# Moved places in the loads and sums, and the order P6, P2, P7, P5 in two groups of an attention and MLP kernel

## The chip, the cores and the metric

One Trainium2 chip, one of its cores. The time is the device time of one execution in microseconds, the median of several executions. The order of work is written out by hand for each engine: SP issues all DMA, TensorE multiplies, ScalarE (ACT), VectorE (DVE) and GpSimd (POOL) prepare operands and empty the accumulators, and semaphores join them.

## What is computed

Four batches of 8 heads, 576 tokens and 64 columns per head. Windowed attention gives x (2304 tokens x 512), a mix of rank 32 over the tokens is added to it, then comes a two layer network with a residual, then a gated layer:

```python
attn = softmax(scale * q @ k.T + bias, window 128) @ v      # per head, joined to x
u  = x + (x.T @ U @ V).T                                    # rank 32 over tokens
x2 = u + relu(u @ w_ch1) @ w_ch2                            # 512 -> 2048 -> 512
h  = relu(x2 @ w_in); a, v = halves of h                    # 512 -> 1024
out = (a * (w_spatial @ norm(v) + b_spatial)) @ w_out       # 512 -> 512
```

## The kernel before

All products are fp32 by parts: each operand is split into a high and a low part (`hi_...` on ScalarE writes a rounded copy, `lo_...` on VectorE or GpSimd the difference), and three matmuls per tile are summed.

The two large products are done block-wise with seven products instead of eight (2 x 2 blocks, sums of blocks as operands). The products are P1 to P7; P1 has blocks 11, P2 blocks 12 and 21, P6, P7, P4 and P5 sums of blocks, P3 a sum on the weights' side. The **up** product (u @ w_ch1) runs in 24 units s = 0 to 23, eight for each of three groups of 768 tokens; in unit s TensorE does P1, P4 and P3 of the unit before, P2, P6, P5, P7 (list `UP`). Of these, `keep_p` on ScalarE copies P1, P6 and P7 to `sums_u`, and `c11`, `c12`, `c22` (VectorE) and `c21` (ScalarE) make the four result blocks, which `store_r` writes to `r_scr`. P3 of a unit can start when `c22` has read P5's bank. At u = 0 and u = 7 of a group, the operands of the next group are made: `x_sum` (sums of blocks of u, on VectorE), `hi_xs` and `lo_xs` (the two parts, `xs`). TensorE needs them in the order 1, 2, 6, 5, 7, 4, 3.

The **down** product (relu(...) @ w_ch2) is a list of 84 entries n (`ENTRIES`): 3 groups g, 7 products, 4 quarters j. Before, the order in each group is P1, then P3 and P4 of the group before, then P2, P6, P5, P7. A ring of three places `rk` holds the operand: `hi_r(n)` on ScalarE waits until entry n - 3 has been used, `lo_r(n)` on VectorE follows, TensorE then does 12 matmuls of 128x384. `r_sum(g, t, j)` on VectorE makes the sums for P7 (t = 3), P6 (t = 2), P4 (t = 4), P5 (t = 1), 16 per group, at places given by the tables `FIRST_T` (group 0) and `NEXT_T`. They read the relu blocks a, b, c, d, which SP reads back from `r_scr` (`load_raw`, `next_raw`). After P1, P6 and P7 ScalarE copies the banks (`keep_dp`) and VectorE adds the residual (`add_res`); `dc` adds P2 (11), P3 (12) and P5 (22), `dc21` adds P4.

VectorE's list over n is, in this order: what ended three entries ago by P2, P3 or P4 gets its `dc`; what ended four entries ago by P1, P6 or P7 gets its `add_res`; and

```python
                if n > RING + 1 and ENTRIES[n - RING - 2][1:] == (7, DP - 1):
                    dc(ENTRIES[n - RING - 2][0], 22)
                lo_r(n)
```

with `dc(g, 22)` waiting for `rk_used` of all of P5 of group g; then the `r_sum` of entry n.

GpSimd splits attention outputs (`lo_x`, tile `xl`) and weights (`split_wc`), and makes the four sums of W1's second pair (`w1_sum_1`, tile `wst`). From the first group change on it makes and splits W2's sums (`split_w2(kk)`, kk = 0 to 7), as soon as the last `lo_xs` of group 1 is done; SP loads them by `W2_LOAD` and stores them by `W2_STORE`, each at a unit s. SP works in strict order, so an issue that waits holds all behind it. The mix of batch 0 (`mix_down`) needs `xl` of pairs 0 to 3.

Of the kernel before, what the change touches and what calls it, by code (L numbers as in the profile page):

```python
# [38 lines left out]
G = 3  # L39
# [46 lines left out]

DN = []
for _g in range(G):
    DN += [(_g, 1)] + ([(_g - 1, 3), (_g - 1, 4)] if _g else []) + [(_g, m) for m in (2, 6, 5, 7)]
# [6 lines left out]
W2_LOAD = {7: [0, 1], 9: [2], 10: [3], 11: [4], 12: [5], 15: [6], 16: [7]}  # L96
# [8 lines left out]
FIRST_T = {(2, 1): [(3, 0), (2, 0)], (2, 2): [(3, 1), (2, 1)], (2, 3): [(3, 2), (2, 2)], (6, 0): [(3, 3), (2, 3)],  # L105
           (6, 1): [(4, 0), (1, 0)], (6, 2): [(4, 1), (1, 1)], (6, 3): [(4, 2), (1, 2)], (5, 0): [(4, 3), (1, 3)]}
NEXT_T = {(4, 1): [(3, 0)], (4, 2): [(3, 1)], (4, 3): [(3, 2), (2, 0)], (2, 0): [(3, 3), (2, 1)], (2, 1): [(2, 2)],
          (2, 2): [(2, 3)], (2, 3): [(4, 0)], (6, 0): [(1, 0), (4, 1)], (6, 1): [(1, 1), (4, 2)],
          (6, 2): [(1, 2), (4, 3)], (6, 3): [(1, 3)]}


def program(nc, qk, v_n, mu, mv, w1, w2, w_in, w_sp, b_sp, w_out, out_t, u_scr, r_scr, w2_scr, x2_scr, wc_scr):
    ctx = ExitStack()
    with ctx:
# [282 lines left out]
        def _(sp):  # L397
# [167 lines left out]
            for p in range(PAIRS, (B - 1) * PAIRS):  # L565
                load_qk(*divmod(p, PAIRS))
                load_v(*divmod(p - 1, PAIRS))
                prepare(p)
            load_qk(B - 1, 0)
# [13 lines left out]
            load_w1(2)  # L583
# [33 lines left out]
            sp.wait_ge(up_p, UP_AT[(NU - 1, 3)])  # L617
# [3 lines left out]
            store_r(NU - 1)  # L621
            load_w2q(5)
# [15 lines left out]
            for g in range(1, G):  # L638
# [10 lines left out]
                if g == G - 1:  # L649
# [3 lines left out]
                    load_group(range(0, WU))  # L653
                store_x2(g, 11)
                if g < G - 1:
                    next_raw(g + 1, "a", 0)
                load_u(g, 21)
                if g < G - 1:
                    next_raw(g + 1, "a", 1)
                    next_raw(g + 1, "b", 0)  # L660
                    next_raw(g + 1, "b", 1)
            sp.wait_ge(rk_lo, ENTRY[(G - 1, 5)] + DP)
            for n in x2_out:
                sp.wait_ge(x2_out[n], 16 * (2 if n != 11 else 3))
            load_x2(0, slice(0, 2), x2_first[0])
            sp.wait_ge(rk_lo, ENTRY[(G - 1, 7)] + DP)
            load_x2(0, slice(2, 3), x2_first[1])
# [6 lines left out]
            sp.wait_ge(rk_used, DN_AT[(G - 1, 7)])  # L674
# [21 lines left out]
        def _(pool):  # L696
# [161 lines left out]
            for p in range(1, (B - 2) * PAIRS + 2):  # L858
# [3 lines left out]
                if p == 2:  # L862
# [34 lines left out]
        def _(act):  # L897
# [227 lines left out]
            for n in range(RING, len(ENTRIES)):  # L1125
# [8 lines left out]
                if g == G - 1 and j == 0 and m == 3:  # L1134
                    act.wait_ge(rk_used, DN_AT[(G - 1, 6)])
# [74 lines left out]
        def _(dve):  # L1210
# [295 lines left out]
            for s in range(1, NU):  # L1506
# [14 lines left out]
                if u == 0:  # L1521
                    lo_xs(g, 5)
                    lo_xs(g, 4)
# [5 lines left out]
                c11(s)  # L1529
                if u == UNITS - 1 and g < G - 1:  # L1530
# [554 lines left out]
```

## Time and profile before

| | us |
|---|---|
| median of 3 runs | 742.55 (742.05 to 748.79) |
| profiled execution, device time | 744.08 |
| its span, first to last instruction | 742.3 |
| TensorE matmuls busy | 721.9 |
| VectorE busy | 455.4 |
| ScalarE busy | 339.3 |
| GpSimd busy | 182.4 |

The profile is of one execution. Its times count from the first instruction. Up products run from 153.3 to 346.6, down products from 340.4 to 525.9 (the last up products lie between its first entries), then the gated layer to the end. Busy TensorE means that a matmul is in flight; matmuls of 384 columns follow each other every 0.173 us. A row of the timeline gives start, duration, engine, line, operation, and in brackets how long the engine stood idle before it and what ended that.

### The profile page before, as it was taken

What the parts mean: (1) busy time and instruction counts of PE and PEld (TensorE: products, weight loads), DVE (VectorE), ACT (ScalarE), POOL (GpSimd) and SP (SyncE); (2) the same over time, 40 slices, a digit from 0 to 9 for tenths busy, and PEclk for the clock granted to TensorE, in tenths of its full rate; (3) what the DMA queues carried; (4) which work ended last, traced back from release to release, by engine and by line L of the source; (5) the groups of instructions that cost most, each with busy time, mean ns of one, the idle gap of its engine ahead of it and who ended that gap; (6) DMA issues with size and microseconds to landing.
All of it is one profiled execution on the core that took longest, in us unless ns stands there. A gap on an engine that the chain in (4) does not pass through costs nothing.

```text
span 742.3 us, 13178 instructions
## 1 busy us (share of the span) xinstructions
PE 721.9 (97%) x4688; PEld 665.2 (90%) x4688; DVE 455.4 (61%) x1032; ACT 339.3 (46%) x764; POOL 182.4 (25%) x183
## 2 busy tenths in 40 slices
PE   8989999989999998999999999999999999999998
PEld 5767777779999998999899999999899998998997
DVE  6858686888855256325977965975466435444431
ACT  5967778855443234224344444444252432432422
POOL 1596645420005884326050000000010100100100
PEclk9999999999999999999999999999999999999999
DMA  6668875045465766797995354645940100100101
GB/s 205 187 236 308 293 261 175 16 142 170 150 216 199 286 245 220 281 346 296 422 304 192 117 167 148 216 163 166 357 167 1 49 17 0 64 0 0 64 0 64
DMA packets 74066, 128.24 MB, mean 173 GB/s; under 512 B 5024, under 2 KB 44960, under 8 KB 73504
## 3 DMA queue, kind: packets, MB, share of 16 engines
q1 hardware_dynamic: 74016, 127.59, 49.7%
q8 instruction: 29, 0.48, 0.3%
q14 instruction: 21, 0.17, 0.1%
HBM read 76.91 MB, written 50.66 MB: 172 GB/s over the span
## 4 chain that ended last, share of the span: by engine, by line
PE 79%; DVE 12%; issue 3%; POOL 2%; ACT 2%; DMA 1%; SPq 0%; DVEq 0%; ACTq 0%; POOLq 0%
PE bank L1862 7%; PE bank L1864 7%; PE bank L1863 7%; PE bank L1704 3%; PE bank L1904 3%; PE wide L1719 3%; PE bank L1905 3%; PE bank L1906 3%; PE bank L2013 2%; PE bank L2015 2%; PE bank L2014 2%; PE bank L1829 2%; PE bank L1827 2%; PE bank L1828 2%; DVE rk L1426 2%
## 5 line engine op out<-in xcount | busy, mean ns | idle before, releaser
L1862 PE MATMUL bank<-xs,w1s 128*128 128x384 f32 x336 | 113.9, 339 | 5.0 <-DVE tok L1416 2.3
L1863 PE MATMUL bank<-xs,w1s 128*128 128x384 f32 x336 | 113.1, 336 | 0.0
L1864 PE MATMUL bank<-xs,w1s 128*128 128x384 f32 x336 | 113.0, 336 | 0.0
L1045 ACT ACTIVATE rk<-tok 128x768 fp32r<-128x768 f32 x72 | 60.8, 848 | 77.5 <-PE bank L1906 34.2
L891 POOL TENSOR_TENSOR vl<-vr,vh 128x512 fp32r<-128x512 f32 x8 | 11.2, 1406 | 296.2 <-ACT vh L1169 296.2
L904 ACT ACTIVATE sc<-sc,mn 128x256 f32<-128x256 f32 (+1 forms) x144 | 67.0, 468 | 20.8 <-DVE mn L1229 20.6
L1028 ACT ACTIVATE sums_u<-bank 128x384 f32<-128x384 f32 x72 | 35.4, 491 | 89.6 <-PE bank L1864 89.3
L1904 PE MATMUL bank<-rk,w2q 128*128 128x384 f32 x208 | 70.6, 339 | 4.0 <-DVE rk L1426 3.0
L1862 PEld LDWEIGHTS bank<-xs,w1s 128*128 128x128 f32 x336 | 63.5, 189 | 7.4 <-DVE tok L1416 2.9
L1905 PE MATMUL bank<-rk,w2q 128*128 128x384 f32 x208 | 69.5, 334 | 0.0
L1906 PE MATMUL bank<-rk,w2q 128*128 128x384 f32 x208 | 69.5, 334 | 0.0
L1864 PEld LDWEIGHTS bank<-xs,w1s 128*128 128x128 f32 x336 | 63.6, 189 | 0.0
L1863 PEld LDWEIGHTS bank<-xs,w1s 128*128 128x128 f32 x336 | 63.6, 189 | 0.0
L1426 DVE TENSOR_TENSOR rk<-tok,rk 128x768 fp32r<-128x768 f32 x48 | 46.6, 976 | 20.6 <-ACT rk L1045 20.4
L1238 DVE COPY pt<-bank 128x512 f32<-128x512 f32 x48 | 31.4, 682 | 24.2 <-PE bank L1704 24.1
L1229 DVE CUSTOM_DVE_ANT_0 sc<-bank,bias 128x256 f32<-128x256 f32 (+1 forms) x128 | 42.3, 384 | 5.4 <-PE bank L1666 3.5
L1904 PEld LDWEIGHTS bank<-rk,w2q 128*128 128x128 f32 x208 | 39.0, 188 | 7.2 <-DVE rk L1426 4.1
L1904 PE MATMUL wide<-rk,w2q 128*128 128x384 f32 x128 | 43.1, 337 | 1.2 <-DVE rk L1426 1.2
L1906 PE MATMUL wide<-rk,w2q 128*128 128x384 f32 x128 | 42.9, 335 | 0.0
L1905 PE MATMUL wide<-rk,w2q 128*128 128x384 f32 x128 | 42.8, 334 | 0.0
L1905 PEld LDWEIGHTS bank<-rk,w2q 128*128 128x128 f32 x208 | 39.1, 188 | 0.0
L1906 PEld LDWEIGHTS bank<-rk,w2q 128*128 128x128 f32 x208 | 39.0, 188 | 0.0
(220 smaller groups left out, 1850.5 us busy)
## 6 DMA issues: line engine op xcount, KB each, us to landing
r_scr<-tok SPq DMA_DIRECT2D x18, 768.0 KB, 4.2
tok<-r_scr SPq DMA_DIRECT2D x18, 768.0 KB, 6.0
qkraw<-qk SPq DMA_DIRECT2D x32, 288.0 KB, 3.9
w1raw<-w SPq DMA_DIRECT2D x32, 256.0 KB, 3.8
w2q<-w_scr SPq DMA_DIRECT2D x4, 2048.0 KB, 13.1
wc_scr<-wprep SPq DMA_DIRECT2D x12, 512.0 KB, 4.0
w_scr<-tok SPq DMA_DIRECT2D x11, 512.0 KB, 3.4
u_scr<-tok SPq DMA_DIRECT2D x6, 768.0 KB, 4.9
```

The costliest lines, as they stand in the source:

```text
L904: act.activation(w, w, ACT.Exp, bias=mn[:, s, n:n + 1], scale=-1.0, accum_out=sm[:, i, c:c + 1]).then_inc(exp_done, 1)
L1028: act.activation(sums_u[:, i, :], a_ps[s % 2][:, 0:HT], ACT.Copy).then_inc(kept, 1)
L1045: act.activation(rk[:, n % RING, 0], raw[RAW_OF[m]][:, 2 * j:2 * j + 2, :], ACT.Relu if m <= 3 else ACT.Copy).then_inc(rk_hi, 1)
L1229: dve.tensor_tensor_reduce(out=out, in0=src, in1=add, scale=-SCALE, scalar=3e38, op0=ALU.add, op1=ALU.min, accum_out=mn[:, s, n:n + 1]).th ...
L1238: dve.tensor_copy(pt[:, f % 2, f // 2 * BANK:(f // 2 + 1) * BANK], pt_ps[f % 2][:, :]).then_inc(pt_kept, 1)
L1426: dve.tensor_tensor(lo, x, hi, ALU.subtract).then_inc(rk_lo, 1)
L1862: pe.matmul(o, wh, ah, start=(k == 0 and m in FRESH), stop=False, skip_group_check=True)
L1863: pe.matmul(o, wl, ah, start=False, stop=False, skip_group_check=True)
L1864: last = pe.matmul(o, wh, al, start=False, stop=(k == 1), skip_group_check=True)
L1904: pe.matmul(o, wh, rh, start=(kk == 0 and m in FRESH), stop=False, skip_group_check=True)
L1905: pe.matmul(o, wl, rh, start=False, stop=False, skip_group_check=True)
L1906: last = pe.matmul(o, wh, rl, start=False, stop=(kk == UNITS - 1), skip_group_check=True)
```

## The change

Six things. The order of P2, P6, P5, P7 in the down product of groups 1 and 2 becomes P6, P2, P7, P5, with one new table of sums for both and one for group 0, whose sums stand one entry earlier. In the up product's group change on VectorE, `c22` moves ahead of `x_sum(4)` and `lo_xs(6)`, and `lo_xs(4)`, `lo_xs(3)` move back by one operation. `w1_sum_1` moves from pair 2 to pair 3, `load_w1(2)` to pair 7. W2's parts 6 and 7 are loaded one unit later. Block c of group 0 is read after P7 instead of P3 of the last unit. The order of SP's loads around the end of a group follows the new order of products.

```diff
+ORDER = {0: (2, 6, 5, 7), 1: (6, 2, 7, 5), 2: (6, 2, 7, 5)}
-    DN += [(_g, 1)] + ([(_g - 1, 3), (_g - 1, 4)] if _g else []) + [(_g, m) for m in (2, 6, 5, 7)]
+    DN += [(_g, 1)] + ([(_g - 1, 3), (_g - 1, 4)] if _g else []) + [(_g, m) for m in ORDER[_g]]
-W2_LOAD = {7: [0, 1], 9: [2], 10: [3], 11: [4], 12: [5], 15: [6], 16: [7]}
+W2_LOAD = {7: [0, 1], 9: [2], 10: [3], 11: [4], 12: [5], 16: [6], 17: [7]}
-FIRST_T = {(2, 1): [(3, 0), (2, 0)], ...
+SUMS = {
+    0: {(2, 0): [(3, 0), (2, 0)], (2, 1): [(3, 1), (2, 1)], ...
+    2: {(4, 1): [(3, 0), (2, 0)], (4, 2): [(3, 1)], (4, 3): [(2, 1), (3, 2)], (6, 0): [(2, 2), (3, 3)],
+        (6, 1): [(2, 3)], (2, 1): [(4, 0)], (2, 2): [(4, 1), (1, 0)], (2, 3): [(4, 2), (1, 1)],
+        (7, 0): [(4, 3), (1, 2)], (7, 1): [(1, 3)]}}
+SUMS[1] = SUMS[2]
@@ sync
                 prepare(p)
+                if p == 7:
+                    load_w1(2)
...
-            load_w1(2)
...
-            sp.wait_ge(up_p, UP_AT[(NU - 1, 3)])
+            sp.wait_ge(up_p, UP_AT[(NU - 1, 7)])
             sp.wait_ge(r_out[0], 16 * NU // 2)
             load_raw(0, "c", 0)
             load_raw(0, "c", 1)
             store_r(NU - 1)
+            sp.wait_ge(up_p, UP_AT[(NU - 1, 3)])
...
+                load_u(g, 21)
                 store_x2(g, 11)
                 if g < G - 1:
-                    next_raw(g + 1, "a", 0)
-                load_u(g, 21)
-                if g < G - 1:
-                    next_raw(g + 1, "a", 1)
                     next_raw(g + 1, "b", 0)
                     next_raw(g + 1, "b", 1)
-            sp.wait_ge(rk_lo, ENTRY[(G - 1, 5)] + DP)
+                    next_raw(g + 1, "a", 0)
+                    next_raw(g + 1, "a", 1)
+            sp.wait_ge(rk_lo, ENTRY[(G - 1, 7)] + DP)
             for n in x2_out:
                 sp.wait_ge(x2_out[n], 16 * (2 if n != 11 else 3))
+            load_x2(0, slice(2, 3), x2_first[1])
+            sp.wait_ge(rk_lo, ENTRY[(G - 1, 5)] + DP)
             load_x2(0, slice(0, 2), x2_first[0])
-            sp.wait_ge(rk_lo, ENTRY[(G - 1, 7)] + DP)
-            load_x2(0, slice(2, 3), x2_first[1])
             sp.wait_ge(rk_used, DN_AT[(G - 1, 5)])
             load_group(range(WU, WO))
...
-            sp.wait_ge(rk_used, DN_AT[(G - 1, 7)])
             load_group(range(WO, WS))
@@ gpsimd
-                if p == 2:
+                if p == 3:
                     w1_sum_1()
@@ scalar
-                    act.wait_ge(rk_used, DN_AT[(G - 1, 6)])
+                    act.wait_ge(rk_used, DN_AT[(G - 1, 2)])
@@ vector
                 if u == 0:
                     lo_xs(g, 5)
-                    lo_xs(g, 4)
...
                 c11(s)
+                if u == 0:
+                    lo_xs(g, 4)
                 if u == UNITS - 1 and g < G - 1:
                     lo_xs(g + 1, 2)
-                    x_sum(g + 1, 4)
-                    lo_xs(g + 1, 6)
...
+                c22(s)
                 if u == 0:
                     lo_xs(g, 3)
-                c22(s)
+                if u == UNITS - 1 and g < G - 1:
+                    x_sum(g + 1, 4)
+                    lo_xs(g + 1, 6)
...
-                for t, k in FIRST_T.get((m, j), []) if g == 0 and m != 4 else []:
-                    r_sum(0, t, k)
                 ahead = g + 1 if m == 4 else g
-                for t, k in NEXT_T.get((m, j), []) if 0 < ahead < G else []:
+                for t, k in SUMS[ahead].get((m, j), []) if ahead < G else []:
                     r_sum(ahead, t, k)
```

**VectorE, change to the next group in the up product, before.** The rows run from `lo_xs(g + 1, 2)` (L1333, tile `xs`) on; L1350 is `x_sum(4)`, L1354 `x_sum(1)`, L1416 `c22`, L1404 and L1410 `c12` with its relu.

```order
L1333 TENSOR_TENSOR xs<-tok,xs 128x768 [waits xs_hi]
L1350 TENSOR_TENSOR tok<-tok 128x2x384 [waits xs_lo,xs_t2,u_out1]
L1333 TENSOR_TENSOR xs<-tok,xs 128x768 [waits xs_hi]
L1416 TENSOR_TENSOR tok<-bank2,sums_u 128x384 [waits r_out1,u3_kept,up_p]
L1354 TENSOR_TENSOR tok<-tok 128x2x384 [waits xs_lo,xs_t4]
L1333 TENSOR_TENSOR xs<-tok,xs 128x768 [waits xs_hi]
L1404 TENSOR_TENSOR tok<-bank2,sums_u 128x384 [waits r_out1,u2_kept,up_p]
L1410 TENSOR_SCALAR tok<-tok 128x384 [waits c12_done]
L1333 TENSOR_TENSOR xs<-tok,xs 128x768 [waits xs_hi] x2
```

And of the changed kernel, from the same instruction on (its lines are six higher, so `c22` is L1422):

```order
L1339 TENSOR_TENSOR xs<-tok,xs 128x768 [waits xs_hi]
L1422 TENSOR_TENSOR tok<-bank2,sums_u 128x384 [waits r_out1,u3_kept,up_p]
L1356 TENSOR_TENSOR tok<-tok 128x2x384 [waits xs_lo,xs_t2,u_out1]
L1339 TENSOR_TENSOR xs<-tok,xs 128x768 [waits xs_hi]
L1360 TENSOR_TENSOR tok<-tok 128x2x384 [waits xs_lo,xs_t4]
L1339 TENSOR_TENSOR xs<-tok,xs 128x768 [waits xs_hi]
L1410 TENSOR_TENSOR tok<-bank2,sums_u 128x384 [waits r_out1,u2_kept,up_p]
L1416 TENSOR_SCALAR tok<-tok 128x384 [waits c12_done]
L1339 TENSOR_TENSOR xs<-tok,xs 128x768 [waits xs_hi]
```

`c22` stands two operations earlier; the number of operations ahead of the split for P5 (the last row) is the same.

**SP, stores and loads of W2's parts 6 and 7, before.** L493 loads two halves of a part (`w1raw`), L499 stores its sums (`w_scr`), L482 stores a unit's result (`r_scr`), and the last row reads relu block a.

```order
L482 DMA r_scr<-tok 512x1x384 [waits c21_done,c22_done,c11_done,r_relu]
L493 DMA w1raw<-w 128x512 [waits w2_sum]
L493 DMA w1raw<-w 128x512
L482 DMA r_scr<-tok 512x1x384 [waits c21_done,c22_done,c11_done,r_relu]
L493 DMA w1raw<-w 128x512 [waits w2_sum]
L493 DMA w1raw<-w 128x512
L482 DMA r_scr<-tok 512x1x384 [waits c21_done,c22_done,c11_done,r_relu]
L499 DMA w_scr<-tok 128x2x512 [waits w2_low] x2
L482 DMA r_scr<-tok 512x1x384 [waits c21_done,c22_done,c11_done,r_relu]
L499 DMA w_scr<-wst 128x2x512 [waits w2_low]
L499 DMA w_scr<-tok 128x2x512 [waits w2_low]
L482 DMA r_scr<-late 128x1536 [waits c21_done,c22_done,c11_done,r_relu]
```

Of the changed kernel, the same piece:

```order
L488 DMA r_scr<-tok 512x1x384 [waits c21_done,c22_done,c11_done,r_relu] x2
L499 DMA w1raw<-w 128x512 [waits w2_sum]
L499 DMA w1raw<-w 128x512
L488 DMA r_scr<-tok 512x1x384 [waits c21_done,c22_done,c11_done,r_relu]
L505 DMA w_scr<-tok 128x2x512 [waits w2_low] x2
L499 DMA w1raw<-w 128x512 [waits w2_sum]
L499 DMA w1raw<-w 128x512
L488 DMA r_scr<-tok 512x1x384 [waits c21_done,c22_done,c11_done,r_relu]
L505 DMA w_scr<-wst 128x2x512 [waits w2_low]
L505 DMA w_scr<-tok 128x2x512 [waits w2_low]
L488 DMA r_scr<-late 128x1536 [waits c21_done,c22_done,c11_done,r_relu]
```

The load of part 7 has moved behind the store of part 6, which waits for GpSimd.

**VectorE, end of a group of the down product, before.** The rows run from the `add_res` after P6 to the end of the `add_res` after P7 and `dc(2, 22)` (L1466 on banks 0 and 1); L1426 is `lo_r` of a sum, L1423 of a block as read.

```order
L1456 TENSOR_TENSOR sums_d<-sums_d,u_in 128x384 [waits du2_kept]
L1426 TENSOR_TENSOR rk<-tok,rk 128x768 [waits rk_hi] x8
L1456 TENSOR_TENSOR sums_d<-sums_d,u_in 128x384 [waits du3_kept,u_back0]
L1456 TENSOR_TENSOR sums_d<-sums_d,u_in 128x384 [waits du3_kept]
L1426 TENSOR_TENSOR rk<-tok,rk 128x768 [waits rk_hi]
L1466 TENSOR_TENSOR sums_d<-bank0,sums_d 128x384 [waits du3_u,rk_used]
L1466 TENSOR_TENSOR sums_d<-bank1,sums_d 128x384 [waits du3_u]
L1423 SCALAR_TENSOR_TENSOR rk<-raw_c,rk 128x768 [waits rk_hi] x2
```

Of the changed kernel, the same place in group 1 (`lo_r` is L1432 and L1429, `dc` L1472, `add_res` L1462):

```order
L1432 TENSOR_TENSOR rk<-tok,rk 128x768 [waits rk_hi] x5
L1462 TENSOR_TENSOR sums_d<-sums_d,u_in 128x384 [waits du3_kept,u_back0]
L1462 TENSOR_TENSOR sums_d<-sums_d,u_in 128x384 [waits du3_kept]
L1432 TENSOR_TENSOR rk<-tok,rk 128x768 [waits rk_hi]
L1472 TENSOR_TENSOR sums_d<-bank0,sums_d 128x384 [waits du3_u,rk_used]
L1472 TENSOR_TENSOR sums_d<-bank1,sums_d 128x384 [waits du3_u]
L1429 SCALAR_TENSOR_TENSOR rk<-tok,rk 128x768 [waits rk_hi] x4
```

`dc(g, 22)` now stands directly ahead of the four splits of the next group's P1, entries 48 to 51, and TensorE's entries before those, 44 to 47, are P5, whose end it waits for.

## Rows read from the trace of the kernel before

**Rows 1.** The page, part 1: busy us, share of the span, instructions.

```profile
PE 721.9 (97%) x4688; PEld 665.2 (90%) x4688; DVE 455.4 (61%) x1032; ACT 339.3 (46%) x764; POOL 182.4 (25%) x183
```

**Rows 2.** Who waited for whom, TensorE: us in total, times, longest.

```profile
PE bank L1904 <- DVE rk L1426: 3.0, 8, 0.9
PE bank L1862 <- DVE tok L1416: 2.3, 2, 1.8
PE wide L1759 <- POOL xl L702: 2.0, 1, 2.0
PE bank L1862 <- ACT sums_u L1028: 1.5, 1, 1.5
...
PE bank L1904 <- issue: 1.0, 1, 1.0
```

**Rows 3.** Stretches: busy us by engine, then TensorE's clock, DMA share, GB/s.

```profile
51.65:55.06 3.41, 3.41 (x10) 2.52 (x9) 0.00 (x0) 0.00 (x0) 3.08 (x3) 0.50 1.06 402
...
283.76:287.17 3.41, 3.41 (x13) 3.41 (x12) 3.38 (x6) 1.22 (x2) 0.00 (x0) 0.50 0.85 287
308.00:344.00 36.00, 36.00 (x210) 36.00 (x209) 13.98 (x22) 11.40 (x22) 15.00 (x14) 1.00 1.02 367
```

**Rows 4.** Timeline of GpSimd and TensorE at the mix of batch 0.

```profile
46.58 0.74 POOL L773 TENSOR_TENSOR wst<-w1raw 128x256 f32<-128x256 f32 x1
...
49.46 1.53 POOL L702 TENSOR_TENSOR xl<-xn,xh 128x640 fp32r<-128x640 f32 x1
...
51.04 0.50 PE L1759 MATMUL wide<-xh,ust 128*128 128x512 f32 x1 [1.98 <-POOL xl L702]
```

**Rows 5.** Timeline of ScalarE and TensorE, unit 0.

```profile
161.84 0.63 ACT L984 ACTIVATE w1s<-w1raw 128x512 fp32r<-128x512 f32 x1 [3.24 <-DMA w1raw<-w]
...
163.21 0.48 ACT L1028 ACTIVATE sums_u<-bank 128x384 f32<-128x384 f32 x1
...
163.75 0.44 PE L1862 MATMUL bank<-xs,w1s 128*128 128x384 f32 x1 [1.47 <-ACT sums_u L1028]
```

**Rows 6.** Timeline of ScalarE, VectorE, TensorE at both group changes.

```profile
218.81 0.49 ACT L1028 ACTIVATE sums_u<-bank 128x384 f32<-128x384 f32 x1 [0.32 <-PE bank L1864]
...
223.83 1.82 DVE L1333 TENSOR_TENSOR xs<-tok,xs 128x768 fp32r<-128x768 f32 x2
...
224.93 0.41 PE L1862 MATMUL bank<-xs,w1s 128*128 128x384 f32 x1 [0.15 <-DVE xs L1333]
...
278.45 1.58 DVE L1333 TENSOR_TENSOR xs<-tok,xs 128x768 fp32r<-128x768 f32 x1
...
282.51 0.45 PE L1862 MATMUL bank<-xs,w1s 128*128 128x384 f32 x1 [1.77 <-DVE tok L1416]
...
284.97 1.82 DVE L1333 TENSOR_TENSOR xs<-tok,xs 128x768 fp32r<-128x768 f32 x2
```

**Rows 7.** SP's issues, landing of unit 22's store at 337.37, VectorE's first sum.

```profile
285.67 1.68 SPq L493 DMA_DIRECT2D w1raw<-w  x2
...
309.52 1.12 SPq L514 DMA_DIRECT2D tok<-r_scr  x2
...
337.37 0.32 SPq L482 DMA_DIRECT2D r_scr<-late  x1
...
r_scr<-late SPq DMA_DIRECT2D x1, 768.0 KB, 8.5
...
346.82 0.92 SPq L514 DMA_DIRECT2D raw_c<-r_scr  x2
...
351.65 0.96 DVE L1435 SCALAR_TENSOR_TENSOR tok<-raw_c,tok 128x768 f32<-128x768 f32 x1 [0.93 <-DMA raw_c<-r_scr]
```

**Rows 8.** Timeline of group 1: VectorE's additions and split, TensorE, ScalarE's copy.

```profile
424.59 1.01 DVE L1466 TENSOR_TENSOR sums_d<-bank,sums_d 128x384 f32<-128x384 f32 x2
...
426.52 0.44 PE L1904 MATMUL wide<-rk,w2q 128*128 128x384 f32 x1 [0.95 <-DVE rk L1426]
...
431.34 0.33 PE L1904 MATMUL bank<-rk,w2q 128*128 128x384 f32 x1
...
431.53 0.87 ACT L1055 ACTIVATE sums_d<-wide 128x384 f32<-128x384 f32 x2 [1.75 <-PE wide L1906]
```

More of the change, by code:

```diff
@@ L103 @@
 WC_STORE = {p + 4: ms for p, ms in WC_AFTER.items()}
[L105 to L109, printed above, removed]
+SUMS = {
[8 rows of a table added]
+SUMS[1] = SUMS[2]
 def program(nc, qk, v_n, mu, mv, w1, w2, w_in, w_sp, b_sp, w_out, out_t, u_scr, r_scr, w2_scr, x2_scr, wc_scr):
```

5 rows, old and new, of the table SUMS are left out of this document.

## The prediction

> **What bounds the kernel now.** First the busy time of the engines over the whole span [rows 1]: TensorE has 721.9 of 742.3 us of matmuls, and VectorE, the next, has 455.4. So a part of the change counts only where TensorE stands still, and what it can give is what the list of TensorE's waits holds [rows 2]: 3.0 us and more on VectorE's `rk` (the second factor of the down products), 2.3 us on its `tok` (the sums of the up products), 2.0 us on GpSimd, 1.5 us on ScalarE, and 1.0 us called issue, which is down product P4 of the last group waiting for a copy. After that the granted clock: it is at its upper level, 2.4 GHz, but for two stretches of 3.41 us at 1.2 GHz [rows 3]. The first follows on the 1.98 us in which TensorE waited for GpSimd [rows 4], the second on a wait of 1.77 us for VectorE [rows 6]; a wait of 1.47 us [rows 5] and all shorter ones were followed by none. A stretch of 3.41 us at half speed does the work of 1.7 us, so it costs 1.7 us. Below I use these times. Down product work comes in entries, a quarter of a product, 12 matmuls, 2.08 us of TensorE.
>
> **Part A, GpSimd's four sums for W1, moved behind p = 3.** The mix of batch 0 starts TensorE again at 51.04, when `xl` of pair 3 is written [rows 4]. The four sums took GpSimd from 46.58 to 49.46, directly ahead of it. Without them `xl` runs from about 46.6 to 48.1, earlier than TensorE arrives (51.04 - 1.98 = 49.06). The 1.98 us go, and with them the cause of the first half-speed stretch: -3.7. Nobody needs the sums before unit 1 of the up product. Bounds: -2.0 (the clock falls anyway) to -3.7; I take -3.7, since the trace has that fall only behind such a wait.
>
> **Part B, load of W1's third pair at p = 7 instead of after the stores of u.** ScalarE stood 3.24 us until 161.84 for it, and only then came to the copy of P7, at 163.21, for which TensorE waited 1.47 us, to 163.75 with a slower first matmul (0.44) [rows 5]. With the data there long before, ScalarE does the split at 158.6, the copy at 160.1, and P4 follows at once: -1.6. Bounds: 0 and -1.6. SP has a free place for two more issues at p = 7, and qk is loaded one step ahead.
>
> **Part C, the up products at the change of token group.** VectorE now does c22 of the last unit ahead of x_sum 4 and lo_xs 6. It doesn't save VectorE an instruction: the split for P5 comes behind the same seven operations. At the first change ScalarE's copy of P7 runs 218.81 to 219.30, so c22 starts at about 219.4, where VectorE had gone on at once before; c22 (0.47), x_sum 4 and lo_xs 6 (0.87 each), a gap of 0.22 for its own result, x_sum 1, lo_xs 7 (0.87), c12 and relu (0.86) end at 224.42, where lo_xs 5 started at 223.83 before [rows 6]. P5 starts 1.10 behind it (223.83 to 224.93), at 225.5, 0.6 later; the wait at P3 has only moved to P5, where it is 1.55 us. lo_xs 3, now behind c22, is 0.3 late as well: +0.9. Ends: 0, and +2.6 if 1.55 us is enough for the clock to fall (1.47 was not, 1.77 was); nearest 1.47, so +0.9. At the second change the same list, stretched by GpSimd's traffic (1.58 for one lo_xs), lets P3 go at 280.6 in place of 282.51, but lo_xs 5 again starts at 285.1 against 284.97, so P5 waits 2.3 us, to 286.2; before, after the half-speed stretch, it began at 287.3. That gains 1.1, and the stretch, which the longer wait brings too, is then paid behind it, +1.7: +0.6, between -1.1 and +0.8.
>
> **Part D, loads at the turn from up to down.** GpSimd's work on W2 begins when the last lo_xs of group 1 is done, about 2 us later. The load of W2's part 6 stands one unit later, and part 7's behind the store of part 6, which waits for GpSimd [order rows of SP]: part 6 now starts where part 7 did, at 285.67, and part 7 has to follow on its load (about 5 us), its split (eight GpSimd operations, 7 to 8 us by the 0.7 and 1.5 us of [rows 4]) and its store, and needs the same again. That ends at about 312, and the reads of relu block a, before at 309.52, come 3 to 6 us later. From 308 to 344 the DMA engines are full (share 1.02) [rows 3], so most of that arrives at the end of this backlog. There stands the store of unit 22: 337.37, 8.5 us to land, 345.9 [rows 7]. The read of block c now needs only this store and P7 of unit 23, not the last product, and that gains 0.9 us at most (346.82 before), 350.7 for the landing instead of 351.6; with 3.8 us of backlog it is 354.5. And the first two r_sum now stand ahead of the split for entry 5, not behind it: VectorE has eight pairs of sums (1.74) and a split (0.87) after each, 2.61 per entry, more than TensorE's 2.08. The chain that had ended in entry 13 now ends in entry 12: landing + 21.2, then 2.1. Entry 13 starts at 374.0 with the landing at 350.7, 377.8 with 354.5, against 373.1: +0.8 to +4.7. I take +2.5, half of the backlog. The wait at entry 5 (2 us or more) may bring a half-speed stretch, hidden since VectorE is behind anyway.
>
> **Part E, the order P6, P2, P7, P5 in groups 1 and 2.** The waits inside the groups, 0.95 us the longest [rows 8], come from VectorE, which has no gap there. It keeps all 16 sums. Worked through entry by entry (0.87 for a sum or split, 0.93 for a pair of half-size additions, ScalarE 0.86 and 0.76 for its copies) the old list gives 1.1 (the recorded 0.95 and a slow first matmul) and 0.5 of delay at two entries; the new one 0.1, 0.6, 0.2, 0.5, 0.5 and 0.6 at six: 0.9 more per group, +1.8.
>
> The larger item is a line that was not changed. `dc(g, 22)` comes five entries behind the end of P7 and adds P5's banks. P5 was over by then; now it is P5's own last entry that goes just before. So VectorE waits at entry 48 (and 76) until TensorE has used everything, does the two additions, and only then splits the entry that TensorE needs next. [rows 8] give the price: an engine starts 0.19 behind TensorE's last matmul (431.34 to 431.53), the additions and the split take from 424.59 to 426.52, 1.93. So +2.1 at each place; at the second the 1.0 us (with its slow start 1.1) for P7's copy goes, since P5 now lies between P7 and P4: +2.1 and +1.0. As recorded, each is an idle time of 1.96 us, between the 1.98 and over the 1.77 that brought half speed: +3.4 for two. Bounds of these 3.4: 0 and 3.4; nearest rows say 3.4. Part E: +1.8 + 3.1 + 3.4 = +8.3.
>
> The rest (W_u and the first x2 loads behind P5 instead of P7, some 8 us later) is hidden: they land over 10 us ahead of their readers, and none of the large waits of [rows 2] is on a weight or on x2.
>
> **Sum.** -3.7 - 1.6 + 0.9 + 0.6 + 2.5 + 8.3 = +7.0 us. The profiled execution took 744.08 us (span 742.3), so 751.1; the median of three before is 742.55, 1.5 lower, and by it 749.5.
>
> **Rivals.** (1) *The clock stays up behind pauses of 2 us.* Place: entries 48 and 76, and P5 at the second change of group. Then 3.4 + 1.7 go and 744.4 is left, no difference. For it: only two falls are on record, a thin basis. Against: both waits of over 1.7 us brought one. The Trainium skill (TensorE: Matmul & The Clock Gate, "HAM oscillation — how this bites in real kernels") warns as a rule only of idle gaps longer than any of these; by it the new waits cost no more than themselves. The trace so far disagrees.
>
> (2) *The DMA backlog reaches VectorE whole.* Place: block c before entry 5. Landing at 354.5, +2.2 on the forecast, 751.7, slower by more than 1%. The point from which it decides is a landing 0.5 us later than the 352.4 I took. For it: DMA share 1.02 over 36 us. Against: small gaps in it before 320 can take up a part.
>
> (3) *The order does what it looks made for.* P6's and P4's waits go (1.6 + 1.6 + 1.1), and the additions find P5 ready. Then -5.3 + 1.5 + 0.8 - 4.3 = -7.3, 735.2. For it: all of the groups' waits do sit at P6 and P4. Against: the order rows of VectorE, in which the additions wait for `rk_used` ahead of the four splits.
>
> **How the numbers follow.** Forecast 0.45, rival (1) 0.22, rival (2) 0.22, rival (3) 0.06, something else 0.05. The forecast's own range is 747.5 to 751.5, so it lies on both sides of +1% (749.98), which is about what a measurement of this kernel can tell from no change. Within 1%: rival (1), over half of the forecast, 0.5. Slower: rival (2), the rest, 0.44. Faster by 1%: 0.06. The range takes in rival (1) and (2) with the upper ends of C: 743.8 to 753.5.
>
> **What would show it.** Right: no wait at the mix of batch 0 and no low clock at 52; P4 of unit 0 without a wait; P3's waits at the changes of group gone and P5's longer; block c landing at 351 to 354 and a wait of 2 us or more at entry 5; two waits of about 2 us for `rk` at P1 of the last group and at its P4, each with 1.2 GHz behind it. Wrong: a whole-kernel clock row without low stretches, or `dc22` not directly behind TensorE's last matmul of P5.

## The result, and the profile after

| | before | after |
|---|---|---|
| median | 742.46 | 751.47 us |
| lowest to highest | 741.43 to 748.79 | 750.63 to 752.87 |
| span of the profiled execution | 742.3 | 749.8 |

The ratio is 1.0108, 95% interval 1.0085 to 1.0132: slower by 1.1%. The forecast was 749.5, range 743.8 to 753.5. The medians are 9.0 apart, the two profiled executions 7.5 (751.58 against 744.08). In experiments 1 and 3 one execution each took far longer than all others (997.75 and 3973.97 us), and the medians given for them leave it out.

The page of the kernel after, part 1, answers to [rows 1]:

```profile
PE 724.5 (97%) x4688; PEld 665.8 (89%) x4688; DVE 455.6 (61%) x1032; ACT 339.1 (45%) x764; POOL 182.9 (24%) x183
```

The instructions and VectorE's busy time are the same; the span grew by 7.5, TensorE's busy time by 2.6. So two thirds are new standing time, and TensorE's waits for whom (us in total, times, longest) say where. They answer to [rows 2]:

```profile
PE bank L1910 <- DVE rk L1429: 6.0, 3, 3.7
PE bank L1910 <- DVE rk L1432: 4.5, 10, 2.1
PE bank L1868 <- DVE xs L1339: 3.6, 2, 2.1
PE bank L1692 <- DVE mn L1235: 2.2, 2, 1.8
```

GpSimd's `xl` and ScalarE's `sums_u` are gone from the list. Waits for `rk` are 11.6 us (6.0, 4.5, and 1.1 at the other banks) in place of 4.2 (3.0 and 1.2), and up product waits are now for `xs`, the split for P5, not for `tok`. The large ones in the timeline (TensorE's first matmul behind each wait; the last bracket is the wait):

```profile
7.83 2.08 PE L1692 MATMUL bank<-qkraw 64*128 64x256 f32 x8 [1.76 <-DVE mn L1235]
...
49.63 0.50 PE L1765 MATMUL wide<-xh,ust 128*128 128x512 f32 x1
...
220.75 0.41 PE L1868 MATMUL bank<-xs,w1s 128*128 128x384 f32 x1 [1.51 <-DVE xs L1339]
...
282.06 0.41 PE L1868 MATMUL bank<-xs,w1s 128*128 128x384 f32 x1 [2.09 <-DVE xs L1339]
...
352.92 0.69 PE L1910 MATMUL bank<-rk,w2q 128*128 128x384 f32 x1 [3.70 <-DVE rk L1429]
...
451.66 0.41 PE L1910 MATMUL bank<-rk,w2q 128*128 128x384 f32 x1 [2.07 <-DVE rk L1429]
...
515.06 0.41 PE L1910 MATMUL bank<-rk,w2q 128*128 128x384 f32 x1 [2.07 <-DVE rk L1432]
```

49.63 is the mix of batch 0, 51.04 with a wait of 1.98 before. The clock by stretches (busy by engine, then TensorE's clock, DMA share, GB/s):

```profile
7.80:11.21 3.41, 3.38 (x15) 2.56 (x16) 1.35 (x9) 2.04 (x9) 0.00 (x0) 0.50 0.62 126
49.00:53.00 4.00, 4.00 (x32) 3.23 (x28) 0.69 (x3) 2.52 (x10) 3.76 (x5) 1.00 1.04 360
282.00:286.00 4.00, 3.94 (x23) 3.97 (x24) 2.23 (x4) 1.07 (x3) 0.00 (x0) 1.00 0.93 285
308.00:344.00 36.00, 35.96 (x207) 35.46 (x206) 14.29 (x22) 11.83 (x22) 16.03 (x16) 1.00 1.00 362
352.50:355.91 3.41, 2.99 (x9) 2.99 (x10) 3.38 (x5) 0.00 (x0) 0.00 (x0) 0.50 1.04 441
451.60:456.00 4.40, 4.34 (x25) 4.37 (x26) 2.61 (x3) 0.94 (x2) 0.00 (x0) 1.00 0.24 87
516.35:519.76 3.41, 3.41 (x12) 3.41 (x12) 1.01 (x2) 0.84 (x1) 0.00 (x0) 0.50 1.01 351
```

Half speed came behind the waits at 7.83, 352.92 and 515.06, and not behind those of 2.09 at 282.06 and 2.07 at 451.66.

**The ledger.** ScalarE's copies (`keep_p` of a unit, `hi_r` of entry n + 3, which waits for the end of entry n) have the same numbers in both kernels, so the difference of their starts, after less before, dates each loss. Below it is called the offset; negative means ahead of the kernel before. What it changed by:

| stretch | forecast | measured |
|---|---|---|
| start, to 15 us | 0 | +0.64 |
| A, mix of batch 0 | -3.7 | -3.63 |
| B, unit 0 | -1.6 | -1.74 |
| C, first change of group | +0.9 | +0.90 |
| C, second change of group | +0.6 | -0.97 |
| D, unit 20 to entry 15 (-4.80 to +0.52) | +2.5 | +5.32 |
| entries 16 to 29 | 0 | -0.15 |
| E, sums of group 1 | +0.9 | +1.08 |
| E, `dc22` at entry 48, with the clock | +2.1 + 1.7 | +2.32 |
| E, sums of group 2 | +0.9 | +1.10 |
| E, `dc22` and P7's copy at entry 76, with the clock | +1.0 + 1.7 | +2.62 |
| sum | +7.0 | +7.5 |

A, B and the first change came out as worked; D is twice its term; the clock fell at other places than forecast.

### The profile page after: what moved, and what is told of

Same layout as the page of the kernel before. It is cut to its first block, busy times and chain, and to the rows that moved or that the text cites. A ratio compares the mean times of both kernels' runs of the same rounds, so it can differ in the third digit from the quotient of the medians.

```text
span 749.8 us, 13178 instructions
## 1 busy us (share of the span) xinstructions
PE 724.5 (97%) x4688; PEld 665.8 (89%) x4688; DVE 455.6 (61%) x1032; ACT 339.1 (45%) x764; POOL 182.9 (24%) x183
## 4 chain that ended last, share of the span: by engine, by line
PE 48%; DVE 10%; issue 2%; DMA 2%; ACT 1%; DVEq 0%; SPq 0%
PE bank L1910 3%; PE bank L1912 3%; PE bank L1911 3%; PE bank L2019 2%; PE bank L2021 2%; PE bank L1868 2%; PE bank L2020 2%; PE bank L1835 2%; PE bank L1833 2%; PE bank L1834 2%; PE bank L1870 2%; PE bank L1869 2%; DVE rk L1432 2%; PE wide L1834 2%; PE wide L1835 2%
## 5 line engine op out<-in xcount | busy, mean ns | idle before, releaser
L897 POOL TENSOR_TENSOR vl<-vr,vh 128x512 fp32r<-128x512 f32 x8 | 11.3, 1407 | 303.0 <-ACT vh L1175 303.0
L1910 PE MATMUL bank<-rk,w2q 128*128 128x384 f32 x208 | 72.1, 346 | 10.6 <-DVE rk L1429 6.0
L1911 PE MATMUL bank<-rk,w2q 128*128 128x384 f32 x208 | 70.5, 339 | 0.0
L1912 PE MATMUL bank<-rk,w2q 128*128 128x384 f32 x208 | 70.5, 339 | 0.0
L1432 DVE TENSOR_TENSOR rk<-tok,rk 128x768 fp32r<-128x768 f32 x48 | 46.1, 975 | 15.3 <-ACT rk L1051 15.2
L1910 PEld LDWEIGHTS bank<-rk,w2q 128*128 128x128 f32 x208 | 39.8, 191 | 15.9 <-issue 6.6
L1912 PEld LDWEIGHTS bank<-rk,w2q 128*128 128x128 f32 x208 | 39.7, 191 | 0.0
L1911 PEld LDWEIGHTS bank<-rk,w2q 128*128 128x128 f32 x208 | 39.6, 191 | 0.0
```

The costliest lines, as they stand in the source:

```text
L1432: dve.tensor_tensor(lo, x, hi, ALU.subtract).then_inc(rk_lo, 1)
L1910: pe.matmul(o, wh, rh, start=(kk == 0 and m in FRESH), stop=False, skip_group_check=True)
L1911: pe.matmul(o, wl, rh, start=False, stop=False, skip_group_check=True)
L1912: last = pe.matmul(o, wh, rl, start=False, stop=(kk == UNITS - 1), skip_group_check=True)
```

## The experiments

**1. `dc(g, 22)` put where P5 now ends.** In groups 1 and 2 it is called three entries behind P5, like the `dc` of P2 and P3:

```diff
                     dc21(g) if m == 4 else dc(g, 11 if m == 2 else 12)
+                if ended[1:] == (5, DP - 1) and ended[0] > 0:
+                    dc(ended[0], 22)
...
-                if n > RING + 1 and ENTRIES[n - RING - 2][1:] == (7, DP - 1):
+                if n > RING + 1 and ENTRIES[n - RING - 2] == (0, 7, DP - 1):
```

> The changed kernel with one edit: in groups 1 and 2, dc(g, 22) is called three entries after the end of P5 (before the splits of entries 50 and 78), as the dc of P2 and P3 are; group 0 is as it was. Theory (a call left in a place that fitted the old order): the waits of 2.07 us at entries 48 (451.7) and 76 (515.1) go, with the half-speed stretch behind the second, so -2.3 and -2.6 as the two traces are apart there: 751.5 becomes 746.6. Rival (the additions cost VectorE the same wherever they stand, and the wait only moves to entry 50 or 52): TensorE shows a wait of 1 to 2 us for rk or for the sums at P3, and the time stays within 1.5 us of 751.5. Second rival (the order by itself is what slows the groups): 749 to 750.

Measured: 745.04 (span of the profile 742.8). VectorE's timeline around entry 48, first in the kernel after, with TensorE:

```profile
449.63 1.02 DVE L1472 TENSOR_TENSOR sums_d<-bank,sums_d 128x384 f32<-128x384 f32 x2 [3.92 <-PE bank L1912]
450.57 2.68 DVE L1429 SCALAR_TENSOR_TENSOR rk<-tok,rk 128x768 fp32r<-128x768 f32 x3
...
451.66 0.41 PE L1910 MATMUL bank<-rk,w2q 128*128 128x384 f32 x1 [2.07 <-DVE rk L1429]
```

and in the experiment:

```profile
447.30 1.83 DVE L1429 SCALAR_TENSOR_TENSOR rk<-tok,rk 128x768 fp32r<-128x768 f32 x2 [2.31 <-ACT rk L1051]
449.05 1.01 DVE L1472 TENSOR_TENSOR sums_d<-bank,sums_d 128x384 f32<-128x384 f32 x2
```

After, VectorE stood 3.92 us with the additions at its head, did them, then split, and TensorE waited for the split. In the experiment two splits lie ahead of the additions, and TensorE has no wait at entries 48, 52, 76 or 80. From entry 44 on the offset to the kernel before goes from +0.74 to +0.58, where after it goes from +1.45 to +7.49. So the unchanged line cost 6.2 us, the largest item of all (6.4 by the medians). My expectation of 4.9 left out that P4's wait for P7's copy (1.0 and a slow first matmul) is then gained: the end of group 2 gives -1.28. Both rivals fall: no wait of 1 us came elsewhere in the groups, and the time is 4 below 749. The order of products without it costs +1.07 and +1.12 for the sums, and gives back 1.28: +0.9.

**2. The two early edits alone**, on the kernel before:

```diff
-                if p == 2:
+                if p == 3:
                     w1_sum_1()
...
                 prepare(p)
+                if p == 7:
+                    load_w1(2)
...
-            load_w1(2)
```

> The kernel before with only two of the edits: GpSimd's four sums at pair 3 and the load of W1's third pair at pair 7. Theory: these two give what the traces showed up to unit 0, -3.6 and -1.7: 742.5 becomes 737.2, and the wait of 1.98 us at the mix of batch 0 goes with its half-speed stretch at 52. Rival (time won early is lost again where DMA or GpSimd set the pace at the turn from up to down products, since those loads do not start earlier): the offset of -5.3 at unit 1 has shrunk by 1 to 3 us by entry 13, and the time is 738.5 to 740.5.

Measured: 738.08, ratio 0.9931 (0.9902 to 0.9959). The offset is -2.98 behind the mix, -4.66 at unit 2, -5.96 behind the second change of group, and -5.72 at the end. Of the early gain 0.2 is lost behind the second change, not 1 to 3; the rival falls. The time is 5.1 below the 743.18 of the kernel before beside this run, where 5.3 was expected. Among the executions with a mean clock of 1.000 the two kernels have medians of 741.3 and 737.7, 3.6 apart: that is the two waits alone, 1.98 and 1.6. The rest of the gain is the half-speed stretch behind the first wait, and not every execution of the kernel before has it. The -1.3 at the second change is no part of the edit. TensorE's wait there was as long as before (1.77 in [rows 6]), and the stretch behind it ran at full clock; first its timeline, then the row of the stretch:

```profile
277.72 0.44 PE L1863 MATMUL bank<-xs,w1s 128*128 128x384 f32 x1 [1.76 <-DVE tok L1417]
```

```profile
277.70:281.70 4.00, 3.82 (x21) 3.53 (x21) 3.97 (x6) 2.13 (x4) 0.00 (x0) 1.00 0.87 263
```

**3 and 4. The turn from up to down.** In the kernel after, one edit each: `W2_LOAD` back to `15: [6], 16: [7]`; or group 0's sums back to their old places, `(2, 1)` to `(5, 0)`.

> The changed kernel with W2's parts 6 and 7 loaded one unit earlier again. The turn from up to down cost 5.2 us. Theory (the loads' backlog reaches VectorE whole, then the sums' place adds 2.1): block c lands some 3 us earlier against TensorE, the wait of 3.70 us for rk at entry 5 (352.9) shrinks to about 1 or less and with it its half-speed stretch, and the time falls by about 3.1: 748.4. Rival (the DMA engines are full anyway from 308 on, and the landing does not depend on where W2's parts stand): the wait at entry 5 stays over 3 us and the time is 751 to 752. Second rival (the stretch at half speed behind the wait is what counts): -4.8, 746.7.

> The changed kernel with the sums of group 0 one entry later again (the old table). VectorE then splits entry 5 ahead of its wait for block c. Theory: the chain of sums and splits ends one entry later, so 2.08 us less is lost: the wait at entry 5 goes, a wait of about 1.6 us comes at entry 6 and further small ones to entry 13, and the time is 749.4. Rival (VectorE only has to work the same sums off behind the same landing, so their place changes nothing): 751 to 752. Second rival (what TensorE does while it waits changes the clock as well; without a wait over 2 us no half speed): 747.5 to 748.

Measured: 748.77 and 748.74. VectorE's first sum, which waits for block c, in the kernel after, then with W2's loads back, then with the sums back:

```profile
350.05 0.96 DVE L1441 SCALAR_TENSOR_TENSOR tok<-raw_c,tok 128x768 f32<-128x768 f32 x1 [3.39 <-DMA raw_c<-r_scr]
```

```profile
346.69 0.96 DVE L1441 SCALAR_TENSOR_TENSOR tok<-raw_c,tok 128x768 f32<-128x768 f32 x1 [1.88 <-DMA raw_c<-r_scr]
```

```profile
348.55 0.96 DVE L1441 SCALAR_TENSOR_TENSOR tok<-raw_c,tok 128x768 f32<-128x768 f32 x1 [2.03 <-DMA raw_c<-r_scr]
```

Two intervals from the same rows and ScalarE's copies separate the causes (us):

| kernel | W2's loads at units | sums of group 0 | end of entry 0 to first sum | first sum to end of entry 13 |
|---|---|---|---|---|
| before | 15, 16 | old | 7.59 | 23.89 |
| after | 16, 17 | one earlier | 10.32 | 26.01 |
| experiment 1 | 16, 17 | one earlier | 10.24 | 26.03 |
| 3 | 15, 16 | one earlier | 7.31 | 26.04 |
| 4 | 16, 17 | old | 9.67 | 23.89 |
| 5 | 15, 16 | old | 7.29 | 23.90 |
| 8, the kernel after again | 16, 17 | one earlier | 10.06 | 26.02 |
| 2 | 15, 16 | old | 7.98 | 23.88 |
| 6 | 15, 16 | old | 7.69 | 23.91 |
| 7 | 15, 16 | old | 7.20 | 23.88 |
| 9 | 15, 16 | old | 7.19 | 23.91 |
| 10 | 14, 15 | old | 7.12 | 23.91 |

The second interval has two values, 23.9 and 26.0, with nothing between. It is VectorE working off 16 sums and the splits, and the place of the sums decides whether that ends before entry 12 or 13: 2.1 us, one entry. The first is the landing: 9.7 to 10.3 with the later loads, 7.1 to 8.0 otherwise. The read of block c without the wait for P3 accounts for 0.3 to 0.8 of that (7.1 to 7.3 against 7.6 to 8.0 in the kernel before and runs 2 and 6).

Only the wait in front of TensorE looks different: 1.11 at entry 5 in place of 3.70 in run 3; in run 4 1.18 at entry 3, none at entry 5 and small ones of 0.7 together behind, where 1.6 was expected at entry 6. The expected falls of 3.1 and 2.1 were both 2.7 by the medians; by the offset from unit 20 to entry 15 the turn costs 1.86 (-4.67 to -2.81) and 2.08 (-5.18 to -3.10) in place of 5.32.

After's 5.32 are 2.7 of landing, 2.1 of the sums' place and 0.45 from unit 22 to the end of entry 0, which runs 3 and 4 did not have; of run 4's gain 0.65 is landing. That is also the distance from its theory, 749.4, to the measured 748.74. The 0.45 belongs to the late transfers too, by two other ways. First, `c11` of unit 22 writes a buffer that an earlier store must have left, and waits for that store:

```profile
329.30 0.56 DVE L1404 TENSOR_TENSOR late<-bank,sums_u 128x384 f32<-128x384 f32 x1 [4.04 <-DMA r_scr<-late]
```

`c22` stands behind it, and TensorE's P3 behind `c22`: 0.13. Second, the first down product waits for `w2q`, a part of W2 that GpSimd splits after its load: 0.32. All profiles with W2's loads at 16 and 17 have the wait of `c11` (after 4.04, run 8 4.39, run 1 3.57, run 4 3.40), the others have none. TensorE lost 0.45 in the kernel after and 0.8 in run 8 before the end of entry 0, and nothing there in runs 1 and 4.

The chain behind the late landing, in the timeline of SP and GpSimd in the kernel after, and then unit 22's store in the list of DMA issues (the last number is the us to landing):

```profile
292.36 2.31 SPq L505 DMA_DIRECT2D w_scr<-tok  x2
294.71 1.36 SPq L499 DMA_DIRECT2D w1raw<-w  x2
...
299.04 0.74 POOL L808 TENSOR_TENSOR wst<-w1raw 128x256 f32<-128x256 f32 x1 [4.78 <-DMA w1raw<-w]
...
306.11 0.38 SPq L505 DMA_DIRECT2D w_scr<-tok  x1
...
333.44 0.32 SPq L488 DMA_DIRECT2D r_scr<-late  x1
344.82 0.92 SPq L520 DMA_DIRECT2D raw_c<-r_scr  x2
```

```profile
r_scr<-late SPq DMA_DIRECT2D x1, 768.0 KB, 11.3
```

Part 7 is loaded at 294.71, behind part 6's stores, and GpSimd waits 4.78 us for it. Its last store is issued at 306.11, where before, with TensorE 4.8 us later, it was 306.74. So against TensorE's work it is 4.2 us late. Everything behind joins full DMA engines (share 1.00 from 308 to 344), and the store of unit 22 took 11.3 us where it took 8.5 [rows 7]. It landed at 344.74, against TensorE 3.6 us later than before. So the stretch of full engines took up 0.6 of the 4.2; in the kernel before the share from 312 to 320 was 0.94, which is room for 0.5. The read of block c waited for that store and is issued at 344.82.

**5. All three put right** (runs 1, 3 and 4 together).

> The changed kernel with three edits put right: dc(g, 22) three entries behind P5, W2's parts 6 and 7 loaded one unit earlier, group 0's sums one entry later. Theory (the three costs add up): from the kernel with dc(g, 22) alone put right, 745.1, the landing of block c takes 2.9 and the sums' place 2.1: 740.1; from the first sum to the end of entry 13 it is 23.9 us (26.0 where the sums stand one entry earlier). Rival (the two repairs at the turn give the same time back, since either removes the long wait at entry 5; each alone took 2.4 to 2.7): 742 to 743. What stays above the kernel with the two early edits alone, 738.1, is then the up products' change of group (about 1.2) and the order of products itself (about 0.9).

Measured: 739.58, where 740.1 was expected; the repairs add up. The offset over the turn is -4.49 to -4.78 and the largest wait left is 2.10 at the second change of group. Its profile had one half-speed stretch, behind that wait. From entry 15 to the end the offset goes from -4.78 to -3.86: the order of products by itself costs 0.9 here too.

**6. The new order at the up product's change of group alone**, on the kernel of run 2 (the diff is that of the change, `lo_xs`, `c22`, `x_sum`).

> The kernel before with the sums for W1 at pair 3, W1's third pair at pair 7, and VectorE's new order at the change of group of the up products; nothing else. Theory: the change of group costs TensorE 0.83 at the first and about 0.35 at the second, against the same kernel without it (738.1, offset of unit 22 to the kernel before -5.96): offset -4.8, 739.3. The gain of 0.97 at the second change that the changed kernel showed is that of a half-speed stretch that the kernel before had there and others did not. Rival (moving c22 ahead is what gained 0.97 there): offset -6 or lower at unit 22, 737 to 738. Second rival (nothing at all): 738.1.

Measured: 738.95, against 738.08 without it. The starts of the two profiles differ by 0.7, so the offsets are read as steps. At the first change it goes from -5.35 to -4.42, +0.93, where run 2 has +0.02. At the second it goes by -0.53, at full clock; in the profiles that have full clock there it goes by -0.33 to -0.97 with the edit (after, runs 1, 3, 4, 6, 8) and by -1.31 and -0.95 without (runs 2, 7). So by the means the edit costs about 0.5 there as well, a rough figure, since the -0.97 with it and the -0.95 without it are the same; 1.4 together, and 0.9 by the medians. The theory's 1.2 lies between. The rival falls: the -0.97 in the ledger is not what moving `c22` gained.

**7. Block c and the last group's order**, on the kernel of run 2: block c as in the change, and `(2, 6, 7, 5)` for the last group with `dc(2, 22)` three entries behind P5.

> The kernel before with the sums for W1 at pair 3, W1's third pair at pair 7, block c read behind P7 of the last unit, and, in the last group alone, the order P2, P6, P7, P5 with dc(g, 22) three entries behind P5. Theory: from 738.1 the read of block c gives 0.3 to 0.7, and P4 of the last group no longer waits for the copy of P7 (1.0 and a slow first matmul): 736.4; no wait at entry 76. Rival (VectorE's additions only come together elsewhere, at P3 of the last group): the 1.1 comes back as waits for rk between entries 76 and 80, and the time is 737.5. Second rival (the read of block c is held by the store of unit 22, not by the product): 737.0.

Measured: 737.61. P4's wait went, but the 1.1 came back. The first rival had its size and the time, and neither rival had its place. TensorE's timeline:

```profile
485.71 0.41 PE L1908 MATMUL bank<-rk,w2q 128*128 128x384 f32 x1 [1.01 <-issue]
```

It is P7's first matmul, behind P6. P1, P6, P7 and P4 of one group accumulate in the same banks, so of these whichever follows another directly waits for ScalarE's copy; here the copy ends at 485.61. The wait is 1.01, as it was at P4. P6, P2, P7, P5 keeps the four of a group apart; in this order the wait has only moved.

**8. The kernel after once more**, one profile, for the clock.

> The changed kernel once more, for the clock alone. In its first profile half speed followed the waits of 1.76 (7.8), 3.70 (352.9) and 2.07 us (515.1), and not those of 2.09 (282.1) and 2.07 (451.7). Theory (whether a wait of about 2 us brings half speed is not fixed by the wait, it differs from one execution to the next): the same waits of 1.7 to 2.1 us, with stretches behind another selection of them, and the time differs by 1.7 for each stretch more or less. Rival (the place or the work before the wait decides): the same three stretches, 751 to 752.

Measured: 750.43 (span 748.7). The stretches of its timeline at the five places:

```profile
7.80:11.21 3.41, 2.33 (x18) 1.71 (x20) 2.30 (x14) 2.99 (x13) 0.00 (x0) 1.00 0.70 178
282.00:286.00 4.00, 3.68 (x21) 3.71 (x22) 2.25 (x5) 1.12 (x3) 0.00 (x0) 1.00 0.86 259
353.00:357.00 4.00, 3.43 (x18) 3.12 (x19) 3.93 (x6) 0.85 (x1) 0.00 (x0) 1.00 1.06 448
451.60:456.00 4.40, 3.91 (x22) 3.94 (x23) 2.73 (x4) 0.85 (x1) 0.00 (x0) 1.00 0.24 89
515.50:520.00 4.50, 4.49 (x26) 4.50 (x27) 2.57 (x3) 0.86 (x2) 0.00 (x0) 1.00 1.00 332
```

The trace of this run has no record of the clock, so the 1.00 in its rows shows nothing; the matmuls do. Those of 256 columns follow each other every 0.427 us before 6.5 us and every 0.209 us from 8 us on, and from there no row of matmuls has the doubled distance (26 in the 4.50 us from 515.50). So there was no stretch at half speed, with waits of 2.07 at entries 48 and 76 as before, and of 2.32 at entry 5, behind one of 1.38 at entry 3. At entry 76 the loss is 1.06 in place of 2.62, so the stretch cost 1.56. The turn cost 5.37 against 5.32 with a stretch in it: there it was hidden behind VectorE's work, as forecast.

**9 and 10.** Run 9 is run 7 without the last group's order; run 10 is run 9 with W2's loads one unit earlier still, `14: [6], 15: [7]`.

> The kernel before with the sums for W1 at pair 3, W1's third pair at pair 7, and block c read behind P7 of the last unit. Theory (the last group's order in the run before gave nothing, since the wait for the copy of P6 or P7 goes to whichever of P6, P7, P4 follows another directly; all that run's gain came from block c): VectorE's first sum starts about 7.2 us after the end of entry 0 and the time is that of that run, 737.4 (737 to 737.8). Rival (that run's order did give something): 738.1, as without the edit of block c.

> The same kernel with W2's parts 6 and 7 loaded one unit earlier than in the kernel before (units 14 and 15). GpSimd stood 7.9 us for part 6. Theory (the DMA backlog sets when block c lands, and it grows and shrinks with these loads; one unit later brought 2.7 to 3.0 us): the first sum starts 1 to 2 us earlier than in the run beside it, at 5 to 6.2 us after the end of entry 0, some of VectorE's small waits at entries 6 to 13 go, and the time falls by 0.7 to 1.7. Rival (block c cannot come earlier, because its read is then held by P7 of unit 23 and its own traffic): the first sum within 0.4 us of the run beside it, the time the same within 0.5. Second rival (GpSimd at work on part 6 during the second change of group slows VectorE's sums there): the wait at P3 grows beyond 1.8 us, and the time rises by 0.5 to 2.

Measured: 737.99 (0.9906, 0.9871 to 0.9941) and 737.55 (0.9901, 0.9866 to 0.9935). Run 9 lies just outside the 737 to 737.8 of its theory and next to its rival, 738.1. The two are nearer to each other than runs of one kernel are, so this decides nothing. Its trace has the 7.19 us from entry 0 to the first sum that run 7 had, and the offset falls by 0.5 over group 0 where run 2's rose by 0.2. By the medians (737.99, and 738.08 in run 2) that gain of block c is not shown. Run 10's first sum comes at 7.12: the rival holds. SP's timeline says why; part 6's load and then its store, in run 9 and in run 10:

```profile
274.98 1.86 SPq L493 DMA_DIRECT2D w1raw<-w  x2
...
288.55 1.71 SPq L499 DMA_DIRECT2D w_scr<-tok  x2
```

```profile
275.72 1.34 SPq L493 DMA_DIRECT2D w1raw<-w  x2
...
289.76 1.71 SPq L499 DMA_DIRECT2D w_scr<-tok  x2
```

The load came no earlier, since it stands behind the stores of part 5, which wait for GpSimd, and the store stands at unit 17 in both. The second rival's wait at P3 did grow, to 2.01, with half speed behind it in this profile; the median shows no loss.

Runs 2, 7, 9 and 10 are all below both kernels, by 0.7 to 1.0% against the kernel before beside them; among them no difference is shown.

## Why the prediction came out as it did

The direction, the time and its place in the range were right: 749.5 for 751.47, ratio 1.009 for 1.011. It was not because every term was, and that it came so close is partly luck.

The 7.0 was worked out on an execution of 744.08 us with two stretches at half speed and then added to a median 1.5 lower. The two profiled executions differ by 7.5, near the sum; the medians differ by 9.0. A counts on the loss of a stretch, 1.7 us, that some executions of the kernel before do not have, so at the median it gives less. That is one part of the 1.5 between 7.5 and 9.0; how large a part no run shows. The sentence that the clock is at its upper level but for two stretches also leaves out the start: there the matmuls run at half speed until 7.27 us, and in the profile after until 4.35.

- **A and B** were right to 0.15 (-3.63 and -1.74), and run 2 gives them alone: 5.1 by the medians. They stay to the end. Of the 3.7, 2.0 is the wait and the rest the stretch behind it.
- **C, first change**, right: +0.90, the wait of 1.55 forecast at P5 is 1.51, without a low clock. **C, second change**: the wait of 2.3 at P5 came as 2.09. The failed part is "the stretch, which the longer wait brings too": it brought none. So -0.97 stands near the lower end, -1.1. Run 6 shows that this is the old kernel's stretch missing, and that the edit by itself costs 0.9 to 1.4 over both changes.
- **D** is the term that was mis-sized: "+2.5, half of the backlog". It measured 5.3, above my upper bound of 4.7. The mechanism was right, and the working up to that bound nearly so. The sums' place is 2.1 (runs 3, 4 and 5), where the working had 23.3 from the landing to entry 13 for 21.5 before, 1.8. The landing is as in rival (2), 354.85 on the old kernel's scale (350.05 + 4.80) where that rival said 354.5. What failed is the choice of half. The for-and-against of rival (2) weighed small gaps in the DMA share before 320 against 36 us at 1.02; the gaps took up 0.6 us of 4.2, not half. Read in shorter pieces, the trace of before showed about that much (0.94 from 312 to 320).
- **E, the sums**: +1.08 and +1.10 for 0.9 each. **`dc(g, 22)`**: the wait of 2.07 for the 2.1 at both places, seen from one line that was not changed, and shown by run 1. Without the clock it cost 2.3 and, with P7's copy given back, 1.06 (run 8).
- **The clock terms**, +3.4 in E and +1.7 in C, all rested on "both waits of over 1.7 us brought one". Of the three forecast stretches one came. Rival (1), at 0.22, was right about that rule as far as it said that such waits need not bring one. The forecast was saved by an error the other way: D gave 2.8 more, the start 0.64, and the two places without their stretch 3.1 less (1.57 and 1.48). Run 8 is the same kernel without any of the three stretches of the first profile, and takes 750.43.

So rivals (1) and (2) both came in part, and that their errors nearly cancel is luck. Rival (3) fell: the waits inside the groups did not go.

## What to carry to other kernels

When a hand-written order of products changes, go through every call whose place is counted from one product and which touches another; here a `dc` that stayed five entries behind P7 cost 6.2 us, 1.6 of it by the clock. Where VectorE works a queue off behind a landing, split the cost in two intervals, the landing against TensorE and the queue from the landing on: each is then one plain number, and edits add. Carry a delay of a load at the head of a stretch of full DMA engines on to its end, less only the gaps that rows show: here 3.6 of 4.2 us arrived. And a sum worked out on one profile belongs to that execution; before it is put on a median, take out of it what not every execution has.

## What was not expected of the hardware

**Half speed is not fixed by the wait.** Over twelve profiles of this family it followed some waits and not others of the same place and length: the second change of group with 1.76 to 1.78 us had it before and in run 9, and not in runs 2 and 7; entry 48 with 2.07 us had it in run 3 and not after, in run 4 and in run 8; entry 76 with the same 2.07 had it after and in runs 3 and 4, not in run 8. The second change with 2.09 or 2.10 had it in run 5 and not after, in run 3 and in run 6. Behind the 1.51 at the first change of group, and behind 1.69 and 1.70 at the second (runs 1, 4 and 8), it never came. The one at entry 76 cost 1.56. Run times of one kernel follow it: of 63 executions of the kernel before that were taken beside the experiments, the 18 with a mean clock of 1.000 have a median of 741.3, 12 with 0.998 have 743.2, 15 with 0.995 have 744.1 and 6 with 0.991 have 748.4. A term for the clock behind a wait of about 2 us is thus a chance of 1.6 us, not a sum. The Trainium skill (TensorE: Matmul & The Clock Gate, section "HAM oscillation — how this bites in real kernels") warns as a rule only of gaps longer than these; there the runs differ, since 1.77 us was enough before and in run 9. What decides between two waits of the same length is not worked out here.

**The start has more than one form.** The clock first rises at 4.35 us in one profile and at 7.32 in another, and the rest goes with that. Where it rose by 5.51 (after, runs 1, 2, 3, 5, 9), TensorE was done earlier with its first matmuls, the first exponentials ran at 6.9 and not at 7.21, and TensorE waited longer at 7.8, the longer the earlier the rise: 1.76 for 4.35, 1.74 for 4.37, 1.54 for 4.80, 1.40 for 5.16, 1.32 for 5.35, 1.24 for 5.51. Behind the three longest waits the clock fell again, and the offset after 15 us was +0.64, +0.62 and +0.29; behind the three others it did not, and the offset was -0.3. Where it rose at 6.45 or later (before, runs 4, 6, 7, 10; in run 8 by the distance of the matmuls), the offset is 0. The kernel after had both forms, in its first profile and in run 8, so the +0.64 in the ledger is no effect of the change. The Trainium skill (TensorE: Matmul & The Clock Gate, section "What's actually happening") says that the point at which the clock rises at the start of a kernel varies from run to run of the same kernel; these profiles agree.
